# Transposes of the expert stage moved from TensorE to VectorE and DRAM, with the two products of a token tile set one tile apart

## The chip, the cores and the metric

The kernel runs on one core of one Trainium2 chip. The metric is the device time of one execution in microseconds (us), taken as the median of several runs. A core has a matrix engine (TensorE, PE in the rows, with its weight loads as PEld), VectorE (DVE), ScalarE (ACT), GpSimd (POOL), SyncE (SP) and sixteen DMA engines. Each engine runs its own list of instructions in order and waits on semaphores. SP, ACT and POOL can start DMAs.

## The reference

Attention without softmax (`kv = k^T v` for each head, `q kv`, then a norm over each head), a feed-forward layer with squared relu, and a layer of eight experts of which each token uses one:

```python
# attention: batch 8, 8 heads, 576 positions, head size 64 -> x: 4608 tokens x 512
kv = einsum('bhsd,bhse->bhde', k, v); o = einsum('bhsd,bhde->bhse', q, kv)
x = o / sqrt(mean(o * o, -1) + 1e-6) * g_norm
# feed-forward: w_in 512 x 2048, w_out 2048 x 512
h = x @ w_in; r = maximum(h, 0.0); x = (r * r) @ w_out
# experts: w_gate 512 x 8, w1 8 x 512 x 1024, w2 8 x 1024 x 512
logits = x @ w_gate + modality_bias[modality_id]
e_idx = argmax(logits, 1); gate_w = softmax(logits)[arange(N), e_idx]
for e in range(8):
    mask = e_idx == e
    h = maximum(x[mask] @ w1[e], 0.0)
    out[mask] = gate_w[mask, None] * (h @ w2[e])
```

For the inputs used, the eight experts get 430, 221, 377, 1576, 354, 1245, 142 and 263 tokens. Of the first 4224 tokens, 388 go to expert 0.

## The kernel before

Every product is made of single-precision parts: each operand is split into a high part, which ScalarE writes, and a low part, which VectorE makes by subtraction, and `product3` and `products` issue three matmuls for high-high, high-low and low-high.

**The groups.** Twelve groups of 384 tokens go through attention and feed-forward (`group` of each engine, up to 997 us). In 16 chunks of each group TensorE alternates a first product (12 matmuls of 384 columns) with a second (9 of 512). Work of the attention of the next group and of the routing of the last one is put between the chunks by the tables `ATTEND`, `ROUTE` and `PREPARE`: a place 2c or 2c + 1 stands after the first or second product of chunk c. Beside that the expert weights are split (`load_piece`, `split_piece`, `store_piece`) and stored as high and low halves in DRAM. The result of a group is stored in `rows`, 516 values for each token: the row, the gate and the token number. `send_ids` writes each token's number into the list of its expert.

**The expert stage.** It works in tiles of 128 tokens of one expert. Expert 0 has `EARLY` = 2 tiles that are filled from the first eleven groups and don't wait for the whole routing; every expert then has as many tiles as its tokens need, at least one. The tiles of an expert run in a loop whose length is read from `tiles_i`. For one tile:

- POOL gathers 128 rows by an indirect DMA (`fetch`), copies them (`pass_rows`), and scatters the finished tile before (`scatter`).
- TensorE transposes the four 128 x 128 blocks of the rows (`transpose_rows`, L758), ScalarE and VectorE take the high and low parts (`x_hi` L955, `x_lo` L1109).
- `hidden` (L813): 2 halves of 12 matmuls of 512 columns into `ps_h`. ScalarE applies relu (L1005). TensorE transposes the relu rows (`transpose_h`, L826, four blocks for each half), and ScalarE and VectorE split them again (`h_hi` L1009, `h_lo` L1224).
- `output` (L813): 24 matmuls of 512 columns into `ps_y`. VectorE scales by the gate (L1239).

The order on TensorE is written out in `tile`: the transposes stand inside the products, so that the product of one tile follows that of the last without a gap of its own.

**Weights.** Each expert has 8 pieces of 1 MB (4 for w1, 4 for w2), in two buffers for even and odd experts. SP loads them (`load_weights`, L389): w1 of expert e when the last `hidden` of expert e - 2 is done, w2 when its last `output` is done. A piece waits for the landing of the piece two before it, so that two are in flight.

## Time and profile before

| | |
|---|---|
| median of 3 runs | 1516.83 us (1510.08 to 1517.85) |
| the profiled execution | 1511.03 us, span of the trace 1509.3 us |
| TensorE busy | 1462.7 us, 97% of the span |
| VectorE, ScalarE, GpSimd busy | 41%, 33%, 24% |
| groups, to 997 us | TensorE 97% to 98% busy |
| start of the expert stage, 997 to 1048 us | TensorE 45 of 51 us busy |
| expert stage from the fourth tile on, 1048 to 1503 us | TensorE busy throughout |

A row of the profile gives the line of the kernel, the engine, the output tile and its inputs. Overlapping matmuls count as one busy stretch, so that the pace is read from the starts of the rows, not from the mean length of one. The idle time of an engine that is not the bound costs nothing.

### The profile page before, as it was taken

The page shows a single profiled execution, that of the slowest core. Times are in us where ns is not written, and L with a number is a line of the kernel's source. Part 1 is how long each engine was busy: PE and PEld are TensorE (multiplying, and loading weights), DVE is VectorE, ACT ScalarE, POOL GpSimd, SP SyncE. Part 2 cuts the span into 40 slices and gives each one's busy share as a digit, 9 for nine tenths or more (in the row PEclk, how much of TensorE's full clock was granted, in tenths as well). Part 3 has the DMA queues.
Part 4 walks back from the last instruction along what each step waited for, and adds up shares of the span by engine and source line. Part 5 has one row for each costly group of instructions (what it writes and reads, how often), then busy time and mean ns, then how long its engine had stood idle before and what let it go on. Part 6 is the DMA issues. An engine that isn't in the chain of part 4 may idle for free.

```text
span 1509.3 us, 25413 instructions
## 1 busy us (share of the span) xinstructions
PE 1462.7 (97%) x8299; PEld 1275.2 (84%) x8300; DVE 625.2 (41%) x1538; ACT 499.2 (33%) x927; POOL 364.4 (24%) x377
## 2 busy tenths in 40 slices
PE   5899999999999999999999999998999999999998
PEld 4689988988998988998988998886888888888886
DVE  2373536445555545453727464432222222222222
ACT  2454333433333433433334333222222222222222
POOL 2452212121312121222222131212222222222221
PEclk8999999999999999999999999999999999999999
DMA  6643565553746463465655364754973112751160
GB/s 148 161 117 128 158 174 165 159 181 93 204 124 213 107 207 111 161 166 165 170 160 173 112 169 158 213 203 160 368 294 130 42 42 102 267 195 45 45 256 21
DMA packets 192776, 236.49 MB, mean 157 GB/s; under 512 B 92287, under 2 KB 107039, under 8 KB 192674
## 3 DMA queue, kind: packets, MB, share of 16 engines
q1 hardware_dynamic: 185122, 215.18, 46.6%
q0 software_dynamic: 7552, 20.03, 4.0%
q8 instruction: 54, 0.88, 0.3%
q14 instruction: 48, 0.39, 0.1%
HBM read 148.14 MB, written 88.07 MB: 157 GB/s over the span
## 4 chain that ended last, share of the span: by engine, by line
PE 82%; DMA 6%; issue 4%; DVE 3%; POOL 2%; ACT 1%; SPq 1%; POOLq 0%; DVEq 0%; ACTq 0%
PE ps_y L813 15%; PE ps_h L813 14%; PE ps_h L632 7%; PE ps_y L632 7%; PE ps_h L634 7%; PE ps_h L633 7%; PE ps_y L634 7%; PE ps_y L633 7%; DMA w_lo<-stage 2%; PE ps_b L698 2%; PE ps_b L720 2%; PE ps_a L670 1%; PE ps_c L758 1%; PE ps_y L826 1%; PE ps_a L826 1%
## 5 line engine op out<-in xcount | busy, mean ns | idle before, releaser
L543 POOL TENSOR_TENSOR stage<-stage,stage_hi 128x512 f32<-128x512 f32 x128 | 166.8, 1303 | 644.1 <-ACT stage_hi L925 564.5
L1206 DVE TENSOR_TENSOR g_sb<-relu_sb 128x384 f32<-128x384 f32 x192 | 132.3, 689 | 381.4 <-ACT relu_sb L982 375.9
L632 PE MATMUL ps_h<-xT_hi,weights 128*128 128x384 f32 x768 | 267.8, 349 | 7.1 <-POOL weights L535 3.4
L634 PE MATMUL ps_h<-xT_hi,weights 128*128 128x384 f32 x768 | 259.1, 337 | 0.0
L633 PE MATMUL ps_h<-xT_lo,weights 128*128 128x384 f32 x768 | 258.3, 336 | 0.0
L632 PE MATMUL ps_y<-weights,g_hi 128*128 128x512 f32 x576 | 234.1, 406 | 0.0
L634 PE MATMUL ps_y<-weights,g_lo 128*128 128x512 f32 x576 | 227.9, 396 | 0.0
L633 PE MATMUL ps_y<-weights,g_hi 128*128 128x512 f32 x576 | 226.5, 393 | 0.0
L982 ACT ACTIVATE relu_sb<-ps_h 128x384 f32<-128x384 f32 x192 | 93.9, 489 | 294.7 <-PE ps_h L634 275.2
L813 PE MATMUL ps_y<-weights,xT_hi 128*128 128x512 f32 x640 | 183.4, 399 | 0.0
L813 PE MATMUL ps_h<-weights,xT_hi 128*128 128x512 f32 x640 | 171.8, 390 | 1.4 <-DVE xT_lo L1109 1.4
L632 PEld LDWEIGHTS ps_h<-xT_hi,weights 128*128 128x128 f32 x768 | 145.1, 189 | 14.0 <-ACT relu_sb L982 5.1
L633 PEld LDWEIGHTS ps_h<-xT_lo,weights 128*128 128x128 f32 x768 | 145.2, 189 | 3.5
L634 PEld LDWEIGHTS ps_h<-xT_hi,weights 128*128 128x128 f32 x768 | 144.5, 188 | 0.0
L925 ACT ACTIVATE stage_hi<-stage 128x512 fp32r<-128x512 f32 x128 | 80.4, 628 | 189.8 <-DMA stage<-in_moe_w 189.3
L813 PEld LDWEIGHTS ps_y<-weights,xT_hi 128*128 128x128 f32 x640 | 120.8, 189 | 25.6
L813 PEld LDWEIGHTS ps_h<-weights,xT_hi 128*128 128x128 f32 x640 | 120.1, 188 | 25.0 <-DVE xT_lo L1109 1.7
L1005 ACT ACTIVATE kv_sb<-ps_h 128x512 f32<-128x512 f32 x80 | 47.8, 598 | 257.8 <-PE ps_h L813 251.2
L634 PEld LDWEIGHTS ps_y<-weights,g_lo 128*128 128x128 f32 x576 | 108.3, 188 | 24.1
L633 PEld LDWEIGHTS ps_y<-weights,g_hi 128*128 128x128 f32 x576 | 108.8, 189 | 18.3
L632 PEld LDWEIGHTS ps_y<-weights,g_hi 128*128 128x128 f32 x576 | 108.8, 189 | 17.4
L1211 DVE TENSOR_TENSOR g_lo<-g_sb,g_hi 128x384 fp32r<-128x384 f32 x192 | 121.1, 631 | 5.0
(169 smaller groups left out, 1695.1 us busy)
## 6 DMA issues: line engine op xcount, KB each, us to landing
stage<-in_moe_w SPq DMA_DIRECT2D x128, 256.0 KB
w_hi<-stage_hi SPq DMA_DIRECT2D x128, 256.0 KB, 2.8
w_lo<-stage SPq DMA_DIRECT2D x128, 256.0 KB, 3.0
weights<-w_hi SPq DMA_DIRECT2D x32, 1024.0 KB, 5.8
weights<-w_lo SPq DMA_DIRECT2D x32, 1024.0 KB, 6.3
rows<-y_sb SPq DMA_DIRECT2D x13, 774.0 KB
k_sb<-in_k SPq DMA_DIRECT2D x60, 144.0 KB, 3.4
v_sb<-in_v SPq DMA_DIRECT2D x30, 288.0 KB, 4.1
```

Source lines behind the costliest of these rows:

```text
L543: pool.tensor_tensor(stage[n % 2][:, :], stage[n % 2][:, :], stage_hi[n % 2][:, :].bitcast(F32), ALU.subtract).then_inc(piece_lo, 1)
L632: pe.matmul(out_ap, lhs[0], rhs[0], start=start, stop=False)
L633: pe.matmul(out_ap, lhs[0], rhs[1], start=False, stop=False)
L634: return pe.matmul(out_ap, lhs[1], rhs[0], start=False, stop=stop)
L698: last = pe.matmul(out_bank[lo:hi, hp * P:(hp + 1) * P], qT_from[:, hp, lo:hi], kv_sb[n][:, hp, :], start=True, stop=True)
L720: last = pe.matmul(ps_b[:, t * E:(t + 1) * E], tile_T[:, k_, :], wg_sb[:, k_, :], start=(k_ == 0), stop=(k_ == KC - 1))
L813: last = pe.matmul(out_ap, lhs[x][:, chunk, :], rhs[w][:, chunk, :], start=(i == 0), stop=(i == 3 * chunks_ - 1))
L925: act.activation(stage_hi[n % 2][:, :], stage[n % 2][:, :], ACT.Copy).then_inc(piece_hi, 1)
L982: act.activation(relu_sb[:, :], ps_h[c % 2][:, 0:GROUP], ACT.Relu).then_inc(h_read, 1)
L1005: act.activation(relu_B[half], ps_h[half][:, :], ACT.Relu).then_inc(relu_done, 1)
L1206: dve.tensor_tensor(g_sb[:, :], relu_sb[:, :], relu_sb[:, :], ALU.mult).then_inc(g_done, 1)
L1211: dve.tensor_tensor(g_lo[c % 3][:, :], g_sb[:, :], g_hi[c % 3][:, :].bitcast(F32), ALU.subtract).then_inc(g_lo_done, 1)
```

## The change

- **Products a tile apart.** TensorE now does `hidden` of tile T + 1 and then `output` of tile T (`hidden_of`, `output_of`). None of the 12 transposes of a tile is left on TensorE.
- **The relu rows** are written by ScalarE in another order of columns (`permuted`), stored in DRAM by ScalarE's queue (`store_h`, 512 pieces of 512 bytes for each half), loaded back with the blocks in other places (`load_h`, 128 pieces of 2 KB), and each 32 x 32 block is turned by one VectorE instruction (`turn_h`). `h_hi` and `h_lo` then read SBUF.
- **The token rows** are gathered in four quarters (`fetch`: four indirect DMAs), and turned in the same way (`turn_x`). Rows are stored in the order of columns that this wants, and `w_gate` is loaded in it.
- **The gate** is multiplied into the rows before they are stored (`scale_rows`, at places 15, 17 and 19 of a group), so `rows` has 512 values and the result is only copied out (`copy_out`). The stored rows leave at chunk 10 in place of 8.
- **Token numbers**: the lists are turned into four source indices and a target index for each token by five small matmuls (`spread_ids`) and VectorE and GpSimd (`take_ids`, `tile`).
- **Tiles**: `EARLY` is 3 and the least number of further tiles, `LEAST`, is 2. The loops over experts are written out.
- **Weights**: a piece waits for the landing of the piece before it, so that one is in flight.

```diff
-EARLY = 2
+EARLY = 3
+LEAST = 2
...
-    PREPARE = [(24, "early", 0), (27, "rows", 0)]
+    PREPARE = [(24, "early", 0), (30, "rows", 0)]
...
+            def load_w1(e):
+                if e > 1:
+                    sp.wait_ge(h_ps, tile_before(sp, e - 1) * 2 + (GROUPS * CH + 2))
+                    sp.sem_inc(passed, 1)
+                for piece in range(4):
+                    if piece:
+                        sp.wait_ge(weights_in[e % 2][piece - 1], filled(e))
+                    elif e > 1:
+                        sp.wait_ge(weights_in[(e - 1) % 2][7], filled(e - 1))
+                    load_weights(e, e % 2, piece)
+            def load_w2(e):
+                if e > 1:
+                    sp.wait_ge(y_ps, tile_before(sp, e - 1) + (GROUPS + 1))
+                    sp.sem_inc(passed, 1)
+                for piece in range(4, 8):
+                    sp.wait_ge(weights_in[e % 2][piece - 1], filled(e))
+                    load_weights(e, e % 2, piece)
...
+            def fetch(T, at):
+                if not isinstance(T, int) or T:
+                    pool.wait_ge(rows_turned, T)
+                    pool.sem_inc(passed, 1)
+                for a_ in range(4):
+                    pool.indirect_dma_start(fetched[:, a_ * P:(a_ + 1) * P], None, rows_dram.rearrange("n (b x) -> (n b) x", b=4),
+                                            bass.IndirectOffsetOnAxis(ap=at[:, a_:a_ + 1], axis=0)).then_inc(row_in, 16)
...
             pe.wait_ge(tiles_done, 1)
-            all_experts(pe, weights_wait, lambda T, e2, n, t: tile(T, n))
+            for e in range(E):
+                n_tiles, previous = tiles_of(pe, e), tile_before(pe, e)
+                for piece in range(4):
+                    pe.wait_ge(weights_in[e % 2][piece], filled(e))
+                hidden_of(previous + 1, e % 2)
+                output_of(previous, (e - 1) % 2 if e else 0)
+                for piece in range(4, 8):
+                    pe.wait_ge(weights_in[e % 2][piece], filled(e))
+                with pe.Fori(1, n_tiles) as t:
+                    hidden_of(previous + t + 1, e % 2)
+                    output_of(previous + t, e % 2)
+            output_of(last_tile(pe), (E - 1) % 2)
...
             def relu(T, half):
                 act.wait_ge(h_ps, T * 2 + (GROUPS * CH + half + 1))
-                act.activation(relu_B[half], ps_h[half][:, :], ACT.Relu).then_inc(relu_done, 1)
+                if not isinstance(T, int) or T:
+                    act.wait_ge(h_out[half], T * 16)
+                act.activation(permuted(relu_B[half]), natural(ps_h[half][:, :]), ACT.Relu).then_inc(relu_done, 1)
...
             def h_hi(T, half):
-                act.wait_ge(hT_ps, T * 2 + (half + 1))
...
+                act.wait_ge(hT_done, T * 2 + (half + 1))
+                act.wait_ge(y_ps, T + GROUPS)
...
+            def tile(previous, e, t, rows=True):
+                T = previous + 1
+                relu(T, 0)
+                store_h(T, 0)
+                relu(T, 1)
+                store_h(T, 1)
+                if rows:
+                    x_hi(T + 1)
+                load_h(previous, 0)
+                load_h(previous, 1)
+                h_hi(T, 0)
+                h_hi(T, 1)
...
+            def scale_rows(r, t):
+                dve.wait_ge(gates_done, r.count(1, 1))
+                dve.tensor_scalar(y_sb[:, t, :], y_sb[:, t, :], gate[:, t:t + 1], None, ALU.mult).then_inc(scaled, 1)
...
-            def tile(T, e2, n, t):
+            def tile(previous, e, t):
+                T = previous + 1
+                turn_x(T + 1)
+                x_lo(T + 1)
+                turn_h(T, 0)
+                turn_h(T, 1)
+                copy_out(previous)
                 h_lo(T, 0)
                 h_lo(T, 1)
```

TensorE, the loop over the tiles of an expert, before: `ps_h` is written by `hidden`, `ps_a` and `ps_y1` with `ident` by `transpose_h`, `ps_c` by `transpose_rows`, `ps_y0` by `output`.

```order
L813 MATMUL ps_h1<-weights1,xT0_hi 128x512 x4
L813 MATMUL ps_h1<-weights1,xT0_lo 128x512
L824 ISA
L826 MATMUL ps_a<-ident,kv_sb0 128x128 [waits relu_done]
L826 MATMUL ps_a<-ident,kv_sb0 128x128 x3
L813 MATMUL ps_h1<-weights1,xT0_lo 128x512
L813 MATMUL ps_h1<-weights1,xT0_hi 128x512 x4
L813 MATMUL ps_h1<-weights1,xT0_lo 128x512 x2
L848 REGISTER_ALU [waits hT_hi_done]
L813 MATMUL ps_y0<-weights1,xT1_hi 128x512 [waits y_by_dve]
```

The same place of the changed kernel:

```order
L839 MATMUL ps_h1<-weights1,xT0_hi 128x512 x4
L839 MATMUL ps_h1<-weights1,xT0_lo 128x512 x2
L839 MATMUL ps_h1<-weights1,xT0_hi 128x512 x4
L839 MATMUL ps_h1<-weights1,xT0_lo 128x512 x2
L868 REGISTER_ALU
L869 ISA [waits y_by_dve]
L839 MATMUL ps_y0<-weights1,xT1_hi 128x512 [waits hT_lo_done]
```

The transposes between the products are gone, and `ps_y0` is now the product of the tile before the one in `ps_h1`.

ScalarE, the same loop, before: `kv_sb` holds the relu rows, `xT1_hi` the high part of the turned ones, `xT0_hi` that of the token rows.

```order
L1005 ACTIVATE kv_sb0<-ps_h0 128x512 [waits h_ps]
L1008 REGISTER_ALU
L1009 ACTIVATE xT1_hi<-ps_a 128x512 [waits hT_ps]
L1004 REGISTER_ALU
L1005 ACTIVATE kv_sb1<-ps_h1 128x512 [waits h_ps]
L1008 REGISTER_ALU
L1009 ACTIVATE xT1_hi<-ps_y1 128x512 [waits hT_ps]
```

And in the changed kernel, where `h_rows` is the DRAM copy and `stage_hi` the loaded one:

```order
L1049 DMA h_rows0<-kv_sb0 128x4x128 [waits relu_done,h_in0]
L1038 REGISTER_ALU
L1041 ACTIVATE kv_sb1<-ps_h1 128x4x4x32 [waits h_out1,h_ps]
L1044 REGISTER_ALU
L1049 DMA h_rows1<-kv_sb1 128x4x128 [waits relu_done,h_in1]
L988 REGISTER_ALU
L989 ACTIVATE xT0_hi<-k_sb1 128x4x128 [waits rows_turned]
L1053 ISA
L1056 ISA [waits h_out0]
L1058 DMA stage_hi0<-h_rows0 128x512 [waits hT_done]
L1056 REGISTER_ALU [waits h_out1]
L1058 DMA stage_hi1<-h_rows1 128x512 [waits hT_done]
```

Four DMAs have come onto ScalarE's list, and it waits there for the landing of each store.

SP, the pieces of one expert, before:

```order
L389 DMA weights0<-w1_lo 128x2x1024 [waits weights_in0_0]
L389 DMA weights0<-w1_lo 128x2x1024 [waits weights_in0_1]
L492 TENSOR_LOAD tiles_i
L492 ISA x2
L472 REGISTER_ALU
L389 DMA weights0<-w2_hi 128x4x512 [waits y_ps,weights_in0_2]
L389 DMA weights0<-w2_hi 128x4x512 [waits weights_in0_3]
```

The same pieces, after:

```order
L418 DMA weights0<-w1_lo 128x2x1024 [waits weights_in0_1]
L418 DMA weights0<-w1_lo 128x2x1024 [waits weights_in0_2]
L313 TENSOR_LOAD tiles_i
L313 ISA x2
L509 REGISTER_ALU
L418 DMA weights0<-w2_hi 128x4x512 [waits y_ps,weights_in0_3]
L418 DMA weights0<-w2_hi 128x4x512 [waits weights_in0_4]
```

Each piece, which waited for the piece two before it, waits for the one before it.

## Rows read from the trace of the kernel before

**Rows 1.** Windows: us, busy time of each engine, granted clock, DMA share.

```profile
20.00:997.00 977.00, 952.83 (x5743) 855.93 (x5742) 491.37 (x1215) 373.40 (x716) 247.81 (x200) 0.99 0.54 157
1020.00:1060.00 40.00, 33.88 (x156) 27.26 (x155) 8.65 (x21) 7.78 (x13) 9.63 (x14) 0.91 0.54 186
1048.10:1503.50 455.40, 455.03 (x2221) 373.68 (x2219) 116.20 (x260) 110.74 (x185) 101.61 (x143) 1.00 0.42 152
```

**Rows 2.** Timeline of TensorE through one tile: start, us, instructions.

```profile
1306.27 1.07 PE L813 MATMUL ps_h<-weights,xT_hi 128*128 128x512 f32 x4
...
1307.63 1.07 PE L813 MATMUL ps_h<-weights,xT_hi 128*128 128x512 f32 x4
...
1310.13 0.60 PE L826 MATMUL ps_a<-ident,kv_sb 128*128 128x128 f32 x4
...
1318.57 1.07 PE L813 MATMUL ps_h<-weights,xT_hi 128*128 128x512 f32 x4
```

**Rows 3.** Page, costliest groups: the relu of the expert stage.

```profile
L1005 ACT ACTIVATE kv_sb<-ps_h 128x512 f32<-128x512 f32 x80 | 47.8, 598 | 257.8 <-PE ps_h L813 251.2
```

**Rows 4.** Timeline of SP's queue: expert weights and the token lists.

```profile
1022.84 0.33 SPq L466 DMA_DIRECT2D stage<-lists  x1
1033.68 1.03 SPq L389 DMA_DIRECT2D weights<-w_hi  x2
1039.52 5.45 SPq L389 DMA_DIRECT2D weights<-w_lo  x2
1054.50 1.01 SPq L389 DMA_DIRECT2D weights<-w_hi  x2
...
1115.97 1.01 SPq L389 DMA_DIRECT2D weights<-w_hi  x2
...
1275.79 1.01 SPq L389 DMA_DIRECT2D weights<-w_hi  x2
1280.66 2.94 SPq L389 DMA_DIRECT2D weights<-w_lo  x2
...
1435.60 1.01 SPq L389 DMA_DIRECT2D weights<-w_hi  x2
```

**Rows 5.** Tile `weights` on SP's queue: issue to landing of its pieces.

```profile
DMA to landing us min/median/max: 4.7/6.0/11.5
```

**Rows 6.** Chain of waits, 939 to 958 us: DMAs of 256 KB, start and us.

```profile
939.61 5.54 DMA w_lo<-stage
...
945.24 4.51 DMA stage<-in_moe_w
...
952.26 3.17 DMA w_lo<-stage
...
955.51 2.68 DMA stage<-in_moe_w
```

**Rows 7.** VectorE's low part of the relu rows: ns min/median/max.

```profile
L1224 DVE TENSOR_TENSOR xT_lo<-ps_a,xT_hi x40: 690/692/693, 1004.1 to 1495.8; 128x512 fp32r<-128x512 f32 x40
```

**Rows 8.** Timeline of TensorE, second tile: wait for the token lists.

```profile
1025.64 0.72 PE L890 MATMUL ps_b<-ident,stage 96*128 96x96 f32 x3 [4.36 <-issue]
...
1026.86 1.20 PE L813 MATMUL ps_y<-weights,xT_lo 128*128 128x512 f32 x2
...
1030.36 1.08 PE L813 MATMUL ps_y<-weights,xT_hi 128*128 128x512 f32 x4
```

**Rows 9.** Timeline of GpSimd: the last group's tokens enter the lists.

```profile
1012.98 1.01 POOL L550 DMA_INDIRECT lists<-sent,entry_i  x1 [22.77 <-DVE token L1178]
```

**Rows 10.** Tile `k_sb` from 1060 us: the gather of a tile's rows.

```profile
L573 POOL DMA_INDIRECT k_sb<-rows,idx x34: 997/1000/1014, 1067.2 to 1471.2; - x34
...
DMA to landing us min/median/max: 3.2/3.4/7.0
```

**Rows 11.** Timeline of the end: last products, last scatter.

```profile
1502.51 0.61 PE L813 MATMUL ps_y<-weights,xT_lo 128*128 128x512 f32 x2
...
1504.80 0.97 POOL L589 DMA_INDIRECT out<-q_sb,meta_i  x1 [11.29 <-DVE q_sb L1239]
```

495 lines of the change are left out of this document (255 added, 240 removed).

## The prediction

> **What bounds the kernel now.** I read three views. The windows first [rows 1]: in the groups TensorE is busy 952.8 of 977 us, in the expert stage from the fourth tile on 455.0 of 455.4 us at the full clock. So TensorE's own list sets the end, and a matmul taken off it shortens the run as long as what took its place comes in time. Then the timeline of TensorE [rows 2]: one tile lasts from 1306.27 to 1318.57, 12.30 us (12.29 over many tiles). Six products take 1.36 us (1306.27 to 1307.63), so a half of a tile, 24 products, takes 5.44 and both 10.88; the other 1.41 us are the three groups of four transposes. Third the queue of SP [rows 4], since it sets when weights are there.
>
> **Tiles.** Relu ran 80 times, two for each tile: 40 tiles [rows 3]. The starts of the weight loads, which follow the last `hidden` of an expert, fit the tokens: expert 2's at 1054.50, expert 4's at 1115.97, expert 5's (which waits for the end of expert 3) at 1275.79, that is 13 tiles of 12.29 later, expert 7's at 1435.60 [rows 4]. Now expert 0 has 3 early tiles and at least 2 more, though 430 - 384 = 46 tokens need one. It gets 5 in place of 4, and the others keep 2, 3, 13, 3, 10, 2, 3: tiles 0 to 40, one more than before.
>
> **The sum** goes against the profiled execution, 1511.0 us (5.8 below the median of the runs shown).
>
> *1. TensorE's list.* Before, hidden(3) starts at 1048.10 and the last product ends at 1503.1 [rows 1, 11]: 455.0 us for 37 tiles. After, 38 `hidden` (3 to 40) and 39 `output` (2 to 40) follow the start of hidden(3): 77 x 5.44 = 418.9. That is **-36.1**; the transposes alone are 37 x 1.41 = 52, the extra tile takes back 10.9 and the output that now stands behind hidden(3) 5.4.
>
> *2. The start of the stage*, 997 us to hidden(3). The relu rows of tile 0 now make a trip through DRAM before output(0); hidden(1) follows hidden(0) at once, and waits for relu, high and low part, about 2 us. On VectorE gate, prefix, the three scalings of the last group and the tile counts are queued behind that trip, so the last tokens, which went to the lists at 1012.98 [rows 9], go some 5 us later, and with them the load of the lists at 1022.84 [rows 4], for which TensorE waits already now [rows 8]. Then tile 3 needs the new tables: matmuls, six VectorE operations, four gathers of 1.00 us of POOL each [rows 10] with about 0.3 between, then turn, high and low part. I make this hidden(3) at 1054 in place of 1048.1: **+6**, bounds 0 and +10.
>
> *3. The tail.* output(40) has no `hidden` before it, only output(39), 5.44 us. The trip of its relu rows takes 9.3 (below), so TensorE waits about 4; copying the index before the last scatter adds 1. **+5**, bounds +3 and +8.
>
> *4. Weights, one piece in flight.* Call p the time from one issue to the next. Count from the start S of hidden(3), at 10.88 a tile. Expert 2's w1 can start when hidden(4) is done, S + 16.3. Its w2 must be there before hidden(8), S + 54.4: TensorE waits 8p - 38.1. Expert 3's eight pieces follow at once, needed before hidden(11), S + 87.0: until there it has waited 16p - 70.7 in all. Then long experts give time, until expert 7: free after hidden(35), needed before hidden(39): 8p - 38.1 again. Together 24p - 108.8. Before, two in flight hide this. What is p? A w1 piece on an idle queue: 1275.79 to 1280.66, 4.87 us; a w2 piece beside a gather: 1033.68 to 1039.52, 5.84 [rows 4]; the least landing is 4.7, the median 6.0 with two in flight [rows 5]. The mean of 4.9 and 5.8 is 5.4. A tile now moves 1.5 MB beside the weights (relu rows 0.5 out and 0.5 back, token rows 0.25, results 0.25) where it moved 0.5; for that I add 0.4: p = 5.8, **+30.4** (8.3 before hidden(8), 13.8 up to hidden(11), 8.3 before hidden(39)). Bounds: 5.0 gives 11.2, 6.3 gives 42.4.
>
> *5. The trip of the relu rows.* From the end of hidden(T) to the start of output(T) TensorE has 10.88 us of other work. The second half's chain: relu 0.8 with its handoff [rows 3], store 3.17, load 2.68 [rows 6], a turn of 128 x 512 (not in the trace; bounds 0.5 and 1.3, taken as VectorE's 0.69 for this shape [rows 7]), `copy_out` 0.75, which stands before `h_lo` on VectorE, `h_lo` 0.69, and 0.5 for handoffs: 9.3. It hides with 1.6 to spare. But these are DMAs on quiet engines. With weights in flight the same store took 5.54 and the same load 4.51 [rows 6]: 13.5, TensorE waits 2.6 a tile. Eight pieces at 5.8 last 46 us; for experts 4, 5 and 6 no weight wait covers that, some 12 tiles. With one piece in flight the engines are free between pieces, so I take a third: 12 x 0.9 = **+11**, bounds 0 and 31. Where TensorE waits for weights the trip is covered.
>
> *6. The clock.* After the wait of 4.36 us eight products took 3.50 us (1026.86 to 1030.36) in place of 1.82, in a stretch with a granted clock of 0.91, which means the lower level, 1.2 GHz, for part of it [rows 1, 8]. 1.7 us for each long wait, three behind hidden(3): **+5**, bounds 0 and 7.
>
> *7. At nothing*: three scalings a group on VectorE (half busy there), permuted writes, 20 tiny DMAs on SP's queue before expert 0's last three pieces (needed 25 us later), the later store of rows, and POOL: five indirect DMAs of 1.3 and two index copies with their handoffs, 9.2 of 10.88 us. If POOL's cover is gone, each us over the tile costs 37.
>
> 1511.0 - 36.1 + 6 + 5 + 30.4 + 11 + 5 = **1532 us**, 1.4% slower.
>
> A rule that speaks against the weight waits stands in the Trainium skill (DMA: Bandwidth & Descriptors, "Anatomy of one DMA"): 2.0 us and bytes/436e3, which makes an estimate of 4.4 us for a piece of 1 MB. By it 8p is under 38.1, both waits vanish, and the sum would be 1502. The least landing in the trace, 4.7 [rows 5], speaks for the rows; what it would mean is rival A.
>
> **The rivals.**
>
> *A, faster: pieces come at p of 4.8 to 5.0 and the trip hides.* Weight waits 6 to 11, relu waits 0 to 2, clock 3, start and tail +8: 1511 - 36 + 8 + 3 + 11 = 1497, at best 1490. For it: 4.87 and the 1.6 us to spare. Against it: w2 pieces at 5.84, and three times the traffic of a tile. It decides at p = 5.2 with relu waits under 3.
>
> *B, no change, 1503 to 1519*: p about 5.4 (20.8) and half the relu waits (5): 1517.
>
> *C, every tile waits for the trip, weights in flight or not.* If store and load with 512-byte pieces take 1.5 us more each, the chain is 12.3. Of the 28 tiles outside the weight waits, 16 then lose 1.4 each (22) and the 12 with weights in flight some 2.7 (33): +55 in place of +11, 1576. For it: VectorE can't turn before both halves are in, and a turn could take 1.3. Against: the 2.68 us load, which this chain repeats exactly.
>
> *D, POOL becomes the bound* through the quarter gathers, 12 us a tile: 37 x 1.1 = 41 more, partly instead of the relu waits: 1560. Against: POOL waited most of each tile for VectorE before. That the change doesn't do what it says I exclude: the order shows no transposes left.
>
> **How the numbers follow.** Forecast (slower, 1519 to 1560) 0.52; A 0.18; B 0.15; C 0.12; D 0.03. From A's upper half to the lower part of C: 1494 to 1568. A measurement here tells about 0.5% from no change: faster 0.18, same 0.15, slower 0.67.
>
> **What would show it.** Tile pitch on TensorE: 10.9 us in expert 3's later tiles with no weights in flight (12.3 or more there: C). Relu activations: 82. hidden(3) near 1054 us. Waits of TensorE for weights before hidden(8), hidden(11) and hidden(39), 8 to 14 us each, and issues of weight pieces 5.4 to 6.2 us apart; under 5.1, A holds. Pitches of 12 to 13 us while pieces of experts 4 to 6 come. POOL idle over a us in each tile, or D. The forecast is wrong if p is under 5.2, or if the contended trip still fits into 10.9 us.

## The result and the profile after

The changed kernel takes 1564.5 us (median; 1561.1 to 1574.3), the kernel before 1517.3 beside it: ratio **1.034**, 95% interval 1.029 to 1.038. The forecast was 1532, +1.4%, in a range of 1519 to 1560. Ratios, here and below, are of fast executions alone; one of the kernel before beside runs 15 and 16, of 5145 us, is left out. The profiled execution took 1562.2 us (span 1560.5) against 1511.0: 51 us to find.

The windows of the changed kernel first, with the columns of [rows 1]:

```profile
20.00:997.00 977.00, 952.46 (x5730) 855.59 (x5729) 503.15 (x1234) 372.27 (x716) 252.27 (x208) 0.99 0.57 155
...
1004.50:1067.50 63.00, 39.67 (x176) 30.92 (x174) 24.09 (x68) 11.98 (x21) 12.52 (x18) 0.83 0.70 212
1067.50:1180.00 112.50, 95.20 (x384) 76.53 (x384) 33.05 (x52) 22.91 (x38) 48.39 (x68) 0.92 0.77 254
1180.00:1316.00 136.00, 133.49 (x577) 109.12 (x578) 54.16 (x84) 36.20 (x60) 67.91 (x96) 0.99 0.65 206
1316.00:1418.00 102.00, 88.66 (x361) 70.65 (x360) 35.57 (x55) 22.77 (x38) 40.17 (x59) 0.93 0.81 270
```

Up to 997 us TensorE is as busy as it was. Then TensorE, busy throughout before, has holes in two kinds of stretch: the start of the stage, and the stretches in which weights are loaded (1067 to 1180, 1316 to 1418, and the last one from 1485), at 254 and 270 GB/s and a granted clock of 0.92 and 0.93. Between them, with few weights moving, it is busy 133.5 of 136 us.

What TensorE waited for, 900 to 1560 us (us in total, times, longest):

```profile
PE ps_y L839 <- DVE xT_lo L1304: 40.3, 16, 5.4
PE ps_h L839 <- DVE xT_lo L1182: 17.3, 3, 14.1
PE ps_b L904 <- DMA stage<-lists: 6.0, 1, 6.0
PE ps_y L667 <- DVE g_lo L1284: 3.0, 1, 3.0
PE ps_h L839 <- DMA weights<-w_lo: 2.6, 1, 2.6
```

L1304 is `h_lo`, the end of the trip of the relu rows; L1182 is `x_lo`. The wait for weights, the largest term of the forecast, is 2.6 us in all. It stands before hidden(11), and it is short only because other waits came first. SP's queue, then TensorE:

```profile
1086.06 5.78 SPq L418 DMA_DIRECT2D weights<-w_hi  x2
...
1131.99 7.26 SPq L418 DMA_DIRECT2D weights<-w_hi  x2
...
1179.90 5.28 SPq L418 DMA_DIRECT2D weights<-w_hi  x2
```

```profile
1180.21 1.80 PE L839 MATMUL ps_h<-weights,xT_hi 128*128 128x512 f32 x4 [2.63 <-DMA weights<-w_lo]
```

These are the first pieces of experts 2, 3 and 4. Each piece is issued when the one before has landed, so the sixteen pieces of experts 2 and 3 take 93.84 us, 5.87 each, and hidden(11) starts 0.3 us after expert 4's first piece is issued, which waits for the same landing. It is 112.6 us behind hidden(3), where eight tiles of 10.88 are 87.0: 25.6 lost. At this pace of the pieces hidden(11) could not have come earlier, so the waits for relu rows before it, 14.8 us, cost nothing of their own.

**The start.** From the timeline of all engines (start, us, instruction, in brackets the idle time and its releaser):

```profile
985.49 5.87 SPq L476 DMA_DIRECT2D early_to<-lists  x16
...
997.87 0.71 DVE L1178 STREAM_TRANSPOSE k_sb<-k_sb 128x512 f32<-128x512 f32 x1 [3.30 <-DMA k_sb<-rows,early_idx]
...
999.89 0.55 DVE L1284 TENSOR_TENSOR g_lo<-g_sb,g_hi 128x384 fp32r<-128x384 f32 x1
...
1000.49 0.79 PE L667 MATMUL ps_y<-weights,g_hi 128*128 128x512 f32 x1 [2.99 <-DVE g_lo L1284]
...
1063.63 0.69 DVE L1310 COPY q_sb<-ps_y 128x512 f32<-128x512 f32 x1 [5.35 <-DMA out<-q_sb,out_idx]
...
1067.58 0.80 PE L839 MATMUL ps_h<-weights,xT_hi 128*128 128x512 f32 x1 [14.05 <-DVE xT_lo L1182]
```

The token rows of tile 0 reach VectorE at 997.87, and the last `g_lo` of the groups is queued behind them; TensorE waits 2.99 us and then runs the last nine products slowly, one in 0.43 us instead of 0.23. hidden(0) starts at 1004.50 instead of 997.09: 7.4 us. The wait and the slow products are 5.1 of them. The last group had also begun 5.4 us later (926.02 against 920.62) and, but for the wait, took 3.1 less. Why it began later is not shown; it begins between 922.4 and 937.2 in the versions of the changed kernel below. From hidden(0) to hidden(3) it takes 63.1 us instead of 51.0. hidden(3) starts at 1067.58 instead of 1048.10.

**The tiles.** With no weights in flight the pitch is 10.88 us, as forecast, from hidden(15) at 1228.91 to hidden(23) at 1315.95. Two tiles from the timeline of all engines, first a quiet one, then one beside expert 6's weights. L1041 is relu, L1049 the store, L1058 the loads, L1299 `turn_h`, L1063 `h_hi`:

```profile
1257.11 0.37 ACTq L1049 DMA_DIRECT2D h_rows<-kv_sb  x1
...
1257.93 2.27 ACTq L1058 DMA_DIRECT2D stage_hi<-h_rows  x2
...
1262.96 0.71 DVE L1299 STREAM_TRANSPOSE tile_T<-stage_hi 128x512 f32<-128x512 f32 x1 [0.90 <-DMA stage_hi<-h_rows]
```

```profile
1367.46 0.38 ACTq L1049 DMA_DIRECT2D h_rows<-kv_sb  x1
...
1368.70 5.89 ACTq L1058 DMA_DIRECT2D stage_hi<-h_rows  x2
...
1379.07 0.71 DVE L1299 STREAM_TRANSPOSE tile_T<-stage_hi 128x512 f32<-128x512 f32 x1 [3.60 <-DMA stage_hi<-h_rows]
...
1379.81 0.63 ACT L1063 ACTIVATE xT_hi<-tile_T 128x512 fp32r<-128x512 f32 x1 [3.60 <-DVE tile_T L1299]
1380.35 0.58 ACT L1041 ACTIVATE kv_sb<-ps_h 128x512 f32<-128x512 f32 x1
...
1381.01 1.22 PE L839 MATMUL ps_y<-weights,xT_hi 128*128 128x512 f32 x2 [4.72 <-DVE xT_lo L1304]
```

From the issue of the second store to the turn of its rows: 5.85 us quiet, 11.61 beside weights. TensorE waits 4.72 us, and the next six products take 2.72 us (to 1383.73) instead of 1.36. And ScalarE has the next relu (1380.35) behind `h_hi`, so the next trip starts late too.

What holds the trip up shows in the bytes that the packets of the trace move, in KB (1000 bytes) per microsecond, by queue (SP's with the weights; ScalarE's, whose 512-byte packets are stores and 2 KB packets loads; GpSimd's):

```
us    weights store load gpsimd
1367        0   257    0      0
1368       73     5    0    102
1369      139     0    0    147
1370      364     3    0     12
1371      372    22    0      0
1372       98   220   30      8
1373        0    15  229    163
1374      114     0    2     86
1375      385     0    0      4
1376      417     0    0      0
1377      131     0  231      0
```

The second store, issued at 1367.46, moves in 1372, when the piece of weights is through. The second load can only be issued after it (1374.2), meets the next piece, and moves in 1377. While a piece flows, the trip moves next to nothing.

### The profile page after: what moved, and what is told of

Read it like the earlier page. It is cut to its first block, busy times and chain, and to the rows that moved or that the text cites. A ratio compares the mean times of both kernels' runs of the same rounds, so it can differ in the third digit from the quotient of the medians.

```text
span 1560.5 us, 25340 instructions
## 1 busy us (share of the span) xinstructions
PE 1449.0 (93%) x7873; PEld 1256.7 (81%) x7873; DVE 702.6 (45%) x1574; ACT 503.0 (32%) x931; POOL 488.0 (31%) x551
## 3 DMA queue, kind: packets, MB, share of 16 engines
q10 hardware_dynamic: 55104, 43.00, 9.0%
## 4 chain that ended last, share of the span: by engine, by line
issue 35%; DMA 24%; PE 23%; POOL 11%; DVE 3%; ACT 2%; ACTq 1%; SPq 1%; POOLq 0%; DVEq 0%
POOL stage L569 8%; DMA lists<-sent,entry_i 8%; PE ps_h L839 7%; PE ps_y L839 7%; DMA stage_hi<-h_rows 6%; DMA h_rows<-kv_sb 5%; DMA stage<-in_moe_w 1%; POOL lists L576 1%; PE ps_y L667 1%; PE ps_h L667 1%; PE ps_y L669 1%; PE ps_y L668 1%; PE ps_h L669 1%; PE ps_h L668 1%; DMA w_lo<-stage 1%
## 5 line engine op out<-in xcount | busy, mean ns | idle before, releaser
L1279 DVE TENSOR_TENSOR g_sb<-relu_sb 128x384 f32<-128x384 f32 x192 | 125.7, 655 | 384.3 <-ACT relu_sb L1016 373.0
L839 PE MATMUL ps_y<-weights,xT_hi 128*128 128x512 f32 x656 | 190.2, 414 | 40.3 <-DVE xT_lo L1304 40.3
L839 PE MATMUL ps_h<-weights,xT_hi 128*128 128x512 f32 x656 | 181.9, 400 | 19.9 <-DVE xT_lo L1182 17.3
L839 PEld LDWEIGHTS ps_y<-weights,xT_hi 128*128 128x128 f32 x656 | 129.7, 200 | 75.1 <-DVE xT_lo L1304 47.6
L601 POOL DMA_INDIRECT k_sb<-rows,idx x156 | 151.2, 969 | 74.9 <-issue 40.0
L839 PEld LDWEIGHTS ps_h<-weights,xT_hi 128*128 128x128 f32 x656 | 126.3, 194 | 47.5 <-DVE xT_lo L1182 16.7
L1284 DVE TENSOR_TENSOR g_lo<-g_sb,g_hi 128x384 fp32r<-128x384 f32 x192 | 130.7, 681 | 5.4 <-issue 0.7
```

The costliest lines, as they stand in the source:

```text
L601: pool.indirect_dma_start(fetched[:, a_ * P:(a_ + 1) * P], None, rows_dram.rearrange("n (b x) -> (n b) x", b=4), bass.IndirectOffsetOnAxis ...
L839: last = pe.matmul(out_ap, lhs[x][:, chunk, :], rhs[w][:, chunk, :], start=(i == 0), stop=(i == 3 * chunks_ - 1))
L1279: dve.tensor_tensor(g_sb[:, :], relu_sb[:, :], relu_sb[:, :], ALU.mult).then_inc(g_done, 1)
L1284: dve.tensor_tensor(g_lo[c % 3][:, :], g_sb[:, :], g_hi[c % 3][:, :].bitcast(F32), ALU.subtract).then_inc(g_lo_done, 1)
```

## Experiments

All times are medians beside the kernel before on the same chip; the ratio is to that. **T**: the trip, held up by weight pieces, is the loss. **L**: loading one piece at a time is. **O**: the trip is too long in any case.

**1. Next to no weights.** For experts 2 to 7 `load_weights` moves 16 of the 2048 columns of a piece, and the products run on what the buffers hold.

```diff
+                if expert_number > 1:
+                    sp.dma_start(weights[n][:, columns].bitcast(F32)[:, 0:16], src.rearrange("e k p f -> p (e k) f")[:, 0, 0:16]
+                                 ).then_inc(weights_in[n][piece], 16)
+                    return
```

> The changed kernel, with every weight piece of experts 2 to 7 cut to 8 KB (64 bytes for each of 128 partitions); the products run on whatever the weight buffers hold, so only the time counts. Theory T (the trip of the relu rows through DRAM is long only while 1 MB pieces of weights are in flight): the 40.3 us of waits of ps_y for the turned relu rows go, and with them the slow stretches; hidden(3) still starts near 1067.6, then 37 tiles of 10.88 us (37.5 x 2 halves: 418.9 us minus what is left out) and a tail of 4: 1562 - 62 = about 1500 us (1495 to 1510). Theory L (the pace of loading, one piece in flight, is the bound): the same 1500, since the loading is gone too. Theory O (the trip is too long by itself, whatever else is in flight): the waits stay, over 1540.

1500.1 us, ratio 0.989 (0.986 to 0.993). TensorE's waits, and one window of it (us, busy, clock, DMA share, GB/s):

```profile
PE ps_h L843 <- DVE xT_lo L1186: 18.7, 3, 14.9
...
PE ps_y L843 <- DVE xT_lo L1308: 4.1, 2, 2.5
```

```profile
1068.00:1180.00 112.00, 112.00 (x491) 0.99 0.49 140
```

O falls: without weights the trip hides in every tile, and TensorE is busy 112.0 of 112.0 us. The 64 us between this and the changed kernel belong to weights and trip together; the start (14.9 us) stays.

**2. Two pieces in flight.**

```diff
...
-                        sp.wait_ge(weights_in[e % 2][piece - 1], filled(e))
+                        sp.wait_ge(weights_in[e % 2][piece - 2], filled(e))
```

> The changed kernel, with two pieces of weights in flight as before the change, in place of one. Theory L: pieces arrive earlier, and the stage gets shorter by the greater part of the waits: 1535 us or less. Theory T: loading was not the bound (2.6 us of waits for weights in the trace of after), and two pieces beside the trip make one trip longer though there are fewer such trips: 1555 to 1580 us, and the waits for the turned relu rows stay at 35 us or more, single ones over 5.4.

1590.5 us, ratio 1.050 (1.046 to 1.054), slower than T had it, and far from L. TensorE's longest wait:

```profile
PE ps_y L839 <- DVE xT_lo L1304: 66.8, 12, 8.4
```

No wait for weights is left; the relu rows wait 66.8 us instead of 40.3. Beside the trip, one in flight is not the loss: two make the trip later still.

**3. No trip.** `turn_h` reads `relu_B` directly; `store_h` and `load_h` are empty, and the blocks stay in the wrong places.

```diff
...
-                dve.transpose(h_turned[half], h_swapped[half]).then_inc(hT_done, 1)
+                dve.transpose(h_turned[half], relu_B[half]).then_inc(hT_done, 1)
```

> The changed kernel without the trip: the relu rows are not stored and loaded, VectorE turns the 32 x 32 blocks straight from ScalarE's tile, so the blocks stay in the wrong places and only the time counts. Everything else, one piece of weights in flight too, is as in the changed kernel. Theory T: the waits for turned relu rows (40.3 us) and the slow stretches behind them go, and the waits for weights that they covered come into sight: at 4.9 us a piece 24 x 4.9 - 108.8 = 9 us, at 5.8 us 30 us: 1515 to 1537 us. Theory L: 1550 us or more. If the two share it, the sum of both waits stays near 40 us and the time above 1545.

1519.5 us, ratio 1.002 (1.000 to 1.004). TensorE's waits:

```profile
PE ps_h L839 <- DMA weights<-w_lo: 16.5, 3, 7.3
...
PE ps_y L839 <- DVE xT_lo L1293: 1.5, 1, 1.5
```

As T had it. The three waits stand before hidden(8), hidden(11) and hidden(39), where the prediction put them, with 4.9, 7.3 and 4.3 us; in the changed kernel waits for relu rows come first and cover them. This run understates what the loading costs there: without the trip's traffic a piece takes 5.3 us, in the changed kernel 5.9.

**4. The lists first.** The loads into `early_from` at chunk 10, those into `early_to` behind the load of the lists.

```diff
-                    if m.c == GROUPS - 1 and c == 11:
+                    if m.c == GROUPS - 1 and c == 10:
...
```

> The changed kernel, with the four loads of the early lists at chunk 10 as before the change, and the sixteen small ones of the target rows taken out of the last group and put behind the load of the lists. If these stood in the way of the rows of tile 0, turn_x(0) comes near 990 instead of 997.9, the wait of ps_y for g_lo (3.0 us) and the slow products behind it go, hidden(0) starts near 997.1 instead of 1004.5, and since the routing of the last group hangs on hidden(0), everything behind moves with it: 1557 us (1555 to 1559). If the start of the stage is bound by something that did not move (the lists, the tables of GpSimd), hidden(3) still starts near 1067 and the time stays at 1564.

1565.7 us, ratio 1.037 (1.032 to 1.043): no gain. Yet the start is as expected: hidden(0) at 996.42, hidden(3) at 1059.39, 8.2 us earlier. Only part of it is the edit's: the last group began 3.1 us earlier (922.96), and it then took 73.5 us instead of 78.5, with no wait for `g_lo`. hidden(40) starts at 1533.63, in the changed kernel at 1532.40.

```profile
PE ps_y L839 <- DVE xT_lo L1304: 49.3, 18, 5.6
```

Nine more us of waits for the relu rows took the gain. **5. The rows first** moves `turn_x(3)` and `x_lo(3)` on VectorE ahead of `copy_out(1)`.

> The changed kernel, with VectorE turning the token rows of tile 3 ahead of the copy of result 1, which waits for scatter 0 behind the gathers of tile 3. If that order holds back hidden(3) (it waited 14.05 us), it starts at the landing of the rows plus 2.1 us, near 1064 instead of 1067.6, and the time falls by 3 to 4 us, to 1558 or 1559. If the rows themselves come last (landing 1065), or a later wait takes the 3 us up, the time stays within 1 us of the changed kernel.

1565.1 us, ratio 1.031 (1.027 to 1.035). The same: hidden(3) at 1063.40, 4.2 us earlier, and 52.2 us of waits for the relu rows. Half of the 4.2 is the edit's: from the last gather of tile 3 to the turn of its rows it is 4.95 us instead of 7.09, and the gathers themselves came 2.05 earlier. hidden(11) still starts 4.2 us earlier (1175.98; in run 4 5.8 earlier, 1174.41). The gain goes between hidden(11) and hidden(35): what TensorE loses there grows from 25.8 us to 35.4, in run 4 to 33.2. Why it grows is not shown.

**6, 7. Another order on ScalarE**, so that a late trip doesn't hold back the next relu; then the same with two pieces in flight. VectorE's order goes with it (`copy_out` and the first `h_lo` ahead of the second `turn_h`), and tile 3's rows come first as in 5.

```diff
...
                 relu(T, 0)
                 store_h(T, 0)
+                h_hi(previous, 0)
                 relu(T, 1)
                 store_h(T, 1)
-                x_hi(T + 1)
+                h_hi(previous, 1)
                 load_h(previous, 0)
+                x_hi(T + 1)
                 load_h(previous, 1)
-                h_hi(T, 0)
-                h_hi(T, 1)
...
```

> The changed kernel, one piece in flight, with another order on ScalarE: relu and store of the first half of tile T + 1 ahead of h_hi of tile T (before, h_hi of tile T stood first, and a late trip held back the next relu and so the next trip), and on VectorE copy_out and h_lo of the first half ahead of turn_h of the second; tile 3's rows are turned ahead of tile 2's relu rows. Theory T with ScalarE's list as the loop that hands a late trip on to the next tile: the trip gets 2.5 to 5 us more, most of the 52 us of waits for the turned relu rows goes, and the waits for weights come out as in the run without the trip (16.5 us) or somewhat larger since the pieces come slower beside the trip: 1525 to 1540 us. If the length of the trip alone counts (waits of 4 to 5.5 us each, 17 times, less 2.5 each): 1545 to 1555 us. If the order does not matter: 1560 or more.

> As the run with the other order on ScalarE, with two pieces of weights in flight. With the trip's new slack of 2.5 to 5 us: if the slack takes up most of the longer trips (waits of up to 8.4 us, 12 of them, in the run with two in flight), there are no waits for weights and 10 to 25 us for the relu rows: 1520 to 1535 us, below the run with one in flight. If the contention is stronger than the slack, 1540 us or more, above it.

1560.6 us (1.030; 1.027 to 1.034) and 1556.7 us (1.030; 1.026 to 1.035). Waits of the first:

```profile
PE ps_h L839 <- DMA weights<-w_lo: 23.8, 3, 10.8
PE ps_h L839 <- DVE xT_lo L1184: 22.8, 12, 11.3
PE ps_y L839 <- DVE xT_lo L1306: 12.4, 34, 2.2
```

The waits for relu rows fell from 40.3 to 12.4 us, and the weights' 23.8 came out. But `h_hi` now stands late even in a quiet tile: its pitch became 11.40, which gives every trip 0.52 us more room and would be 19 us over 37 tiles; up to hidden(11) it costs nothing, since the pieces set that start here too (1180.20, where the next piece is issued at 1179.90). Run 7 waits for no weights and 31.6 us for relu rows, in 38 waits of up to 3.0. It was expected at 1520 to 1535, or slower than run 6, and is neither. My expectations had left the pitch out, so these two runs don't tell what the hand-on through ScalarE's list is worth.

**8. One transfer instead of two.** The relu rows go from ScalarE's tile straight into the one that VectorE turns.

```diff
...
-                act.dma_start(h_dram[half].rearrange("a p r -> p a r"),
-                              relu_B[half].rearrange("p (a r) -> p a r", a=4)).then_inc(h_out[half], 16)
+                for a_ in range(4):
+                    act.dma_start(h_swapped[half][a_ * QUAD:(a_ + 1) * QUAD, :],
+                                  relu_B[half][:, a_ * P:(a_ + 1) * P]).then_inc(h_in[half], 16)
...
```

> The changed kernel, one piece of weights in flight, with the relu rows sent from ScalarE's tile straight into the tile that VectorE turns (four DMAs of 128 pieces of 512 bytes for each half), in place of a store to DRAM and a load from it. The output is that of the reference. Theory T: the trip loses one of its two transfers, 2.7 us where it is quiet and about 5.5 us beside a piece of weights, so the contended chain falls from 13.5 to about 9 us, under the 10.88 us of a tile: the waits for the turned relu rows fall from 40 us to under 10, and the waits for weights that they covered appear as in the run without the trip (16.5 us): 1520 to 1535 us. If the 512-byte pieces beside 2 or 4 KB pieces are the slow part of the trip (a store's time, not a load's), the transfer that is left is the slow one and the waits fall by less than half: 1540 us or more.

1577.2 us, ratio 1.038 (1.035 to 1.041), a miss. Waits:

```profile
PE ps_h L839 <- DVE xT_lo L1178: 51.7, 37, 15.4
PE ps_h L839 <- DMA weights<-w_lo: 13.2, 3, 7.7
PE ps_y L839 <- DVE xT_lo L1300: 5.0, 4, 2.7
```

The relu rows wait only 5.0 us, as T said. But 37 times TensorE now waits for the token rows, in quiet tiles too (ScalarE's timeline):

```profile
1289.12 2.52 ACTq L1050 DMA_DIRECT2D stage_hi<-kv_sb  x4
1291.75 0.63 ACT L989 ACTIVATE xT_hi<-k_sb 128x512 fp32r<-128x512 f32 x1 [2.82 <-issue]
```

Four issues take 2.52 us of ScalarE's list, ahead of `x_hi`; the pitch is 11.51. **9** put two pieces in flight and the edits of 4 and 5 on top of it.

> As the run with the direct exchange, and with two pieces of weights in flight, the early lists loaded at chunk 10 with the sixteen small loads behind the load of the lists, and tile 3's rows turned ahead of the copy of result 1. From the run with few bytes of weights (1500 us) the earlier hidden(0) takes 8 us and the earlier hidden(3) 3 us: 1489, plus what waits are left for the relu rows beside two pieces in flight, 0 to 20 us, and none for weights: 1490 to 1510 us, below the kernel before. If two in flight lengthen the one transfer as they lengthened the two (waits of up to 8.4 us, 66.8 us in all): 1520 us or more, above the direct exchange with one in flight.

1585.6 us, ratio 1.042 (1.037 to 1.047), the same list with 48.0 us for token rows and 25.3 for relu rows: a miss too.

**10. Larger packets.** The store writes the relu rows as they lie, in packets of 2 KB; the blocks come back in the wrong places.

```diff
-                act.dma_start(h_dram[half].rearrange("a p r -> p a r"),
-                              relu_B[half].rearrange("p (a r) -> p a r", a=4)).then_inc(h_out[half], 16)
+                act.dma_start(h_dram[half].rearrange("a (x b) r -> (a x) (b r)", b=4), relu_B[half]).then_inc(h_out[half], 16)
```

> The changed kernel, with the relu rows stored as they lie (128 pieces of 2 KB for each half in place of 512 pieces of 512 bytes), so the blocks come back in the wrong places and only the time counts. If the small pieces are what the weights hold up (each waits its turn behind pieces of 2 or 4 KB), the contended store falls from about 5.5 us to 3 and most of the waits for the relu rows go: 1520 to 1540 us. If bytes and the transfer's fixed time count, not the number of its pieces, the time stays within 8 us of 1564.

1572.0 us, ratio 1.036 (1.032 to 1.040), where the changed kernel has 1.034: no difference. The number of the store's packets is not the cause. Of the waits, 27.2 us are for relu rows and 14.5 for weights: 41.7 together, in the changed kernel 42.9.

**11, 12. The direct exchange in a better place.** `x_hi` ahead of the second four issues, the edits of 4 and 5, and one or two pieces in flight.

```diff
...
                 relu(T, 1)
+                x_hi(T + 1)
                 store_h(T, 1)
-                x_hi(T + 1)
...
```

> The direct exchange with one piece of weights in flight, the early lists at chunk 10 and tile 3's rows turned ahead of copy 1 as before, and on ScalarE x_hi of the next tile ahead of the four issues of the second half. In the first run of the direct exchange those four issues (2.53 us) stood ahead of x_hi, and every tile took 11.51 us in place of 10.88, also with no weights in flight. If that is all of its loss: hidden(3) near 1059, then 37 tiles of 10.88 and 16.3 us of outputs, 26 us of waits for weights and slow products as in the run without the trip, 5 to 10 us for the relu rows, 9 us to the end: 1515 to 1528 us. If ScalarE's list is too full of issues in any order (pitch of the quiet tiles still over 11.2): 1540 us or more.

> The same with two pieces of weights in flight. No waits for weights; the relu rows wait 10 to 25 us in all, since one transfer is held up in place of two: 1500 to 1520 us, below the run with one in flight. If two pieces in flight cost the trip more than one in flight costs in waits for weights (as they did with the trip through DRAM, 1590 against 1565): above the run with one in flight, 1530 or more.

1546.4 us (1.022; 1.018 to 1.026) and 1558.2 us (1.028; 1.026 to 1.030), both slower than expected. The quiet pitch is 10.88 again, and hidden(3) starts at 1054.04. In the first:

```profile
PE ps_y L839 <- DVE xT_lo L1300: 26.1, 13, 3.9
PE ps_h L839 <- DMA weights<-w_lo: 19.5, 4, 13.7
```

45.6 us together. So the 5.0 us of run 8 were probably low because its tiles were stretched by the token rows; at the full pace one transfer beside weights is too late as well, only less. Two in flight again costs more than it saves (46.8 us for relu rows, none for weights). Run 11 is 18 us faster than the changed kernel, but most of that is the start: in the profiled executions hidden(3) comes 13.5 us earlier, and behind it run 11 loses 64.6 us where the changed kernel loses 66.6. Against run 4, with the same early lists, which loses 74.8, the single transfer saves 10.

**13, 14. Small parts.** A piece of 1 MB comes as four DMAs of 256 KB, three in flight; first in the changed kernel, then in run 11. Theory F: a trip waits for the piece ahead of it, so its size counts. Theory S: trip and weights share, and the size does not count.

```diff
+                for j in range(4):
+                    before_ = ((e - 2) * 8 + piece) * 4 + j - DEPTH
+                    if before_ >= 0:
+                        sp.wait_ge(*part_in(2 + before_ // 32, before_ // 4 % 8, before_ % 4))
...
+                    sp.dma_start(weights[e % 2][:, at:at + 512].bitcast(F32), part).then_inc(part_in(e, piece, j)[0], 16)
```

> The changed kernel, with each 1 MB piece of experts 2 to 7 loaded by four DMAs of 256 KB (512 of the 2048 columns for every partition), three of them in flight. Theory F (a DMA of the trip that is issued while a piece flows moves nothing until the piece is through, 2.6 us at some 400 KB a microsecond, and the two transfers in a row that hang on each other meet one piece after another): the longest hold-up is now 0.75 MB, 1.9 us, and the rate is about 4.3 us a megabyte (three parts of 2.8 us and 0.4 us of issue in flight), so there are no waits for weights: 1525 to 1545 us. Theory S (trip and weights share the engines by bytes, whatever the size of a DMA; the sum of the waits for relu rows and for weights stays where all runs with the trip had it, 42 to 46 us with one piece in flight and 67 with two): 1560 to 1590 us.

> The same parts of 256 KB, three in flight, with the direct exchange of relu rows, the early lists at chunk 10 and tile 3's rows first. Theory F: one transfer that waits 1.9 us at most, which the slack of a tile takes up: under 10 us of waits for the relu rows and none for weights: 1495 to 1515 us, at or below the kernel before. Theory S: 1545 to 1565 us, as with pieces of 1 MB (1546 with one in flight, 1558 with two).

1567.4 us (1.035; 1.031 to 1.040) and 1542.6 us (1.018; 1.012 to 1.024). F falls for the trip of two transfers. In the first the packets do interleave (weights 133 and 92 KB in 1123 and 1124 us beside 146 and 197 of the store), the longest wait is 4.0 us instead of 5.4, and there are more of them:

```profile
PE ps_y L864 <- DVE xT_lo L1337: 41.4, 18, 4.0
```

41.4 us and none for weights: nearly the sum of before. With the single transfer (run 14) the waits are 21.3 and 11.3 us, 32.6 together against 45.6 in run 11, the least of all, but the times differ by 3.8 us only, within their intervals. In the profiled executions the last group of run 14 begins 14.8 us later than that of run 11 (937.2 against 922.4) and hidden(3) 13.3 later, while behind hidden(3) it loses 48.8 us instead of 64.6. So with the single transfer small parts do help the expert stage, by 16 us, and the groups before it take most of that back. Whether the edit makes the groups longer is not shown. It falls short of what F had said for it as well, under 10 us of waits for relu rows and none for weights.

**15. The rest of the change alone.** No trip (as in 3), two pieces in flight, the edits of 4 and 5. **16. The serial loading alone**, in the kernel before.

> The changed kernel without the trip (the blocks stay in the wrong places), two pieces of weights in flight, the early lists at chunk 10 and tile 3's rows first. It gives what the rest of the change is worth when the exchange of blocks costs no transfer: hidden(3) near 1056, 37 tiles of 10.88 and 16.3 us of outputs, 9 us to the end, and no waits for weights: 1484 to 1495 us, which is 20 to 30 below the kernel before. If two pieces in flight hold up the gathers of the token rows too, or weights are still waited for, 1505 or more.

1487.4 us, ratio 0.983 (0.978 to 0.987). TensorE waits for nothing from hidden(3), at 1054.51, to hidden(40) at 1460.02, 37 tiles of 10.96 on the mean. This is 26 us below the kernel before. Behind hidden(3) it loses 4.9 us, run 3 with one piece in flight 25.8, so one in flight costs 21 us even without the trip.

> The kernel before, with one piece of weights in flight in place of two and nothing else changed. Its tiles are longer (12.3 us against 10.88), so ten of them give 14 us more for 24 pieces. At 5.0 to 5.6 us a piece, read from the run without the trip, its waits for weights come to 0 to 11 us: 1517 to 1530 us. If one in flight costs it nothing, within 3 us of the kernel before, then that part of the change is free by itself.

1560.4 us, ratio 1.030 (1.025 to 1.035).

```profile
PE ps_h L813 <- DMA weights<-w_lo: 32.3, 4, 13.8
...
PE ps_c L758 <- POOL k_sb L582: 5.6, 1, 5.6
```

A miss, by 30 us: I had carried over ten tiles of cover. The kernel before waits for all eight pieces ahead of an expert's first `hidden` (L903), the changed one for the last four only a tile later. Its two longest waits are before the first tiles of experts 2 and 7. So the serial loading is dear where nothing else changes, some 45 us. That the lead which the change gives to w2 is worth a good part of it is argued from this, not tested.

None of these versions with the reference's output is faster than the kernel before.

Where the time behind hidden(3) is lost, in the profiled executions, in us beyond the products' own 5.44 a half:

| run | hidden(3) starts | to hidden(11) | hidden(11) to hidden(35) | behind hidden(35) | sum |
|---|---|---|---|---|---|
| changed kernel | 1067.6 | 25.6 | 25.8 | 15.2 | 66.6 |
| 2, two in flight | 1068.8 | 37.0 | 32.1 | 21.2 | 90.3 |
| 3, no trip | 1065.4 | 16.6 | 1.4 | 7.8 | 25.8 |
| 4 | 1059.4 | 28.0 | 33.2 | 13.6 | 74.8 |
| 5 | 1063.4 | 25.5 | 35.4 | 14.5 | 75.4 |
| 10 | 1072.2 | 26.2 | 23.9 | 15.7 | 65.8 |
| 11 | 1054.0 | 27.9 | 21.8 | 14.9 | 64.6 |
| 13 | 1074.3 | 22.6 | 27.0 | 12.9 | 62.5 |
| 14 | 1067.3 | 20.6 | 15.6 | 12.6 | 48.8 |
| 15, no trip, two in flight | 1054.5 | 3.0 | 0 | 1.9 | 4.9 |

In the changed kernel and in runs 3, 5, 6, 8, 10 and 11, all with one piece in flight, hidden(11) starts 0.3 us after the piece that waits for the sixteenth landing is issued.

## Why the prediction was wrong

Its sum against the profiled execution, 1562.2: -36.1 for the list, +19.5 up to hidden(3) (predicted 6), +66.6 from there to the last product (1067.58 to 1553.1 for 418.9 us of products), +1.2 behind it. Terms 3 to 6 had 51.4 for the last two. By stretch, the forecast's terms give 25.5 us up to hidden(11) (weights 22.1, clock 3.4), 11 to hidden(35), 10.0 to hidden(39) and 4 from there to the last product; measured are 25.6, 25.8, 10.9 and 4.3. So of the 30 us that were missing, 13.5 are in the start and 14.8 between hidden(11) and hidden(35), where the trip alone was priced.

*1, TensorE's list: right.* 82 relus, 41 tiles, a pitch of 10.88. Run 15 shows what it is worth, 26 us below the kernel before with the longer start and the extra tile paid.

*2, the start: mis-sized, 12.1 from hidden(0) to hidden(3) instead of 6.* The last tokens went to the lists at 1027.39, 14.4 us later than in [rows 9] and 7.0 of that after taking off the later hidden(0), where I had 5; the lists' load followed at 1038.22. Behind the tables came what I had not counted: `copy_out(1)` waiting for scatter 0, which stands behind the gathers of tile 3 on GpSimd (5.35 us, ahead of `turn_x(3)`; the edit of run 5 took 2.1 off).

*7, at nothing: wrong by 5.1 of the 7.4 us at hidden(0).* "20 tiny DMAs on SP's queue" were priced against the weights behind them. The first four are themselves what GpSimd's gather of tile 0 waits for, at chunk 11 instead of 10; the gather is now four, and on VectorE the turned rows stand ahead of the last `g_lo`. Run 4 moves the loads, and this wait is gone. The rest is the later start of the last group, whose cause is not shown, so that the scalings and the later store cost nothing is not shown either. POOL holds up no tile: the quiet pitch is 10.88.

*4, weights: the pace right, covered by another wait.* In the changed kernel the pieces follow each other 5.87 us apart up to hidden(11) and 5.4 for expert 7, where I had 5.8. That is partly luck, since both rows that gave it had two pieces in flight. Up to hidden(11) the loading sets the time, as forecast, although TensorE's waits name the relu rows for 14.8 us of it and weights for 2.6. Before hidden(39) it does not: the last piece is issued at 1510.81, hidden(39) starts at 1521.52, and what is lost are 7.5 us of waits for relu rows and slow products, so that 10.9 stands beside 10.0 there is luck. In run 3, without the trip, a piece takes 5.3 us (42.6 for eight, 1084.01 to 1126.61), 24 x 5.3 - 108.8 = 18.4, and the waits are 16.5. The 0.4 that I added for the traffic of a tile was there: 0.6 a piece up to hidden(11), 0.2 for expert 7 (5.4 against 5.2 in run 3).

*5, the trip: the step that failed, 11 instead of 25.8.* The 11 us were for the tiles beside the pieces of experts 4 to 6, between hidden(11) and hidden(35). There TensorE waits 15.6 us for relu rows, and the slow products behind the waits make it 25.8. The pitch from hidden(22) to hidden(29) is 13.7 us, where I had 12 to 13. The quiet chain was right: it hides, and with few weights the waits are 4.1 us (run 1). Rival C's 1576 is nearer to the time than 1532, but its mechanism, every tile waiting, is not there. The contended chain was read from a store and a load of 5.54 and 4.51 us beside other 256 KB transfers [rows 6], and I took a third of the excess because "with one piece in flight the engines are free between pieces". The rows after show the opposite at 1367 to 1377 us: a piece blocks the trip while it flows, and since the load can't be issued before the store has landed, one trip meets two pieces, 11.61 us in place of 5.85. The relu rows also wait where I had only the weights waiting: 14.8 us before hidden(11) and 7.5 before hidden(39). Up to hidden(11) the trip costs by slowing the pieces instead: 25.6 us are lost there, in run 3 16.6. And the row at 1380.35 shows how a late trip delays the next.

*6, the clock: 5 predicted.* Of the 66.6 us, 42.9 are waits for relu rows and weights, so 23.7 are slow products and small gaps: there were 17 waits to fall behind, not three. The stretches have a granted clock of 0.92 and 0.93, the lower level of 1.2 GHz for part of them.

The rule of the Trainium skill that stood against the weight waits (DMA: Bandwidth & Descriptors, "Anatomy of one DMA") gave an estimate of 4.4 us for a piece, and the sum 1502. The page fits it to DMAs that GpSimd issues, and these pieces are issued by SP. For them it does not hold in the trace: 4.7 is the least landing, and pieces one after the other are 5.3 us apart in run 3.

**In one line:** the change takes 36 us from TensorE's list and would gain 26 net if the exchange of blocks cost no transfer and two pieces were in flight (run 15); the exchange and the weights together cost more than that. Which of the two TensorE waits for can be shifted, the sum hardly: 42.9 us in the changed kernel, 41.7, 45.6 and 41.4 in runs 10, 11 and 13, 49.3 and 53.5 in 4 and 5; only run 14 has less, 32.6. One reason is in the table above: with one piece in flight and the trip, sixteen pieces in a row hold hidden(11) 26 to 29 us late, whichever wait comes first. What the trip loses between hidden(11) and hidden(35) does move, from 15.6 us in run 14 to 35.4 in run 5, and why stays open, as does why the two queues don't share while a piece flows.

## What to carry to other kernels

Before moving a step from a compute engine to a round trip through DRAM, look at what else the DMA engines carry while it runs, and price the trip as if each of its transfers, one after the other, waits out a whole transfer of the bulk load (here 11.6 us instead of 5.9). A wait that hides another is no saving: take the candidates away one at a time, as in runs 1, 3 and 15, before believing that a term is small, and look at when the bulk load ends: loads that follow each other without a pause set the time, whatever wait the profile names. And give an engine's issues of DMAs their length in its list: four of them, 2.5 us, ahead of a 0.6 us step cost every tile 0.6.

## What was not expected of the hardware

- A store of 256 KB on ScalarE's queue moved 3 to 22 KB a microsecond while a 1 MB piece on SP's queue moved 364 to 372; the two did not share evenly. With parts of 256 KB they did (146 beside 133 in run 13), and the changed kernel was no faster.
- Pieces of 1 MB, each issued when the one before has landed, came 5.3 us apart without the trip (run 3) and 5.9 beside it (the changed kernel, experts 2 and 3).
- Packets of 2 KB in place of 512 bytes for the stores (23616 packets on that queue in place of 55104) left the time where it was (ratios 1.036 and 1.034).
- A turn of 128 x 512 single-precision values in 32 x 32 blocks on VectorE takes 0.71 us, about as long as a copy of the same shape out of `ps_y` (0.65).
- A DMA from one tile of SBUF into other partitions of another costs ScalarE 0.63 us an issue in a row of four, where a single one to DRAM costs 0.38.
